# Attention and two MLPs in one program: pooled heads in pairs, two of VectorE's sums on GpSimd, and the attention's tasks at other places

## The reference

```python
def _attn_ref(q, k, v):                      # B, H, S, D = 4, 8, 576, 64
    q_d, k_d, v_d = means of q, k, v over each 4 rows         # 144 pooled rows
    out_d = sm_attn(q_d, k_d, v_d)           # softmax(q k / sqrt(D)) v, all 144 x 144
    out_up = np.repeat(out_d, 4, axis=2)
    mask = np.abs(pos[:, None] - pos[None, :]) < 4            # a band of 7 keys
    out_local = softmax(where(mask, q k / sqrt(D), -1e9)) v
    return out_up + out_local

x = attn.transpose(0, 2, 1, 3).reshape(2304, 512)
h = x @ w_in                                 # 512 x 2048
x = (maximum(h, 0) ** 2) @ w_out             # 2048 x 512
h = maximum(maximum(x @ w1, x @ w2), x @ w3) # 512 x 768 each
out = h @ w_out2                             # 768 x 512
```

## Time and profile before

| | |
|---|---|
| device time, median of 3 runs | 857.37 us (855.84 to 858.9) |
| profiled execution, device time | 856.62 us |
| its span | 854.9 us, mean granted clock 0.985 |
| TensorE matmul, weight load | 815.8 us (95%), 783.1 us (92%) |
| VectorE | 447.9 us (52%) |
| ScalarE | 331.6 us (39%) |
| GpSimd | 228.2 us (27%) |

### The profile page before, as it was taken

How to read it: one execution, slowest core, us unless ns; L and a number is a source line. 1 busy time by engine, 2 the same in 40 slices (tenths; PEclk the granted TensorE clock), 3 DMA queues, 4 the chain that set the end, 5 groups by cost and what they waited for, 6 DMA issues and landing times.

```text
span 854.9 us, 13859 instructions
## 1 busy us (share of the span) xinstructions
PE 815.8 (95%) x5701; PEld 783.1 (92%) x5701; DVE 447.9 (52%) x537; ACT 331.6 (39%) x908; POOL 228.2 (27%) x203
## 2 busy tenths in 40 slices
PE   8999979999989998999979999999999999999996
PEld 7888868999979998989979999999999999999996
DVE  5657856859977899767880008721222222122211
ACT  4685454464654454644635344211211112121111
POOL 8476911344411364332433222100000000000000
PEclk9999989999999998999999999999999999999998
...
GB/s 182 277 230 77 49 55 2 16 93 20 102 28 3 40 92 120 30 1 15 30 28 1 1 115 174 75 101 1 38 37 38 38 1 75 1 38 1 20 18 37
DMA packets 52752, 49.06 MB, mean 57 GB/s; under 512 B 23401, under 2 KB 44681, under 8 KB 51921
## 3 DMA queue, kind: packets, MB, share of 16 engines
...
## 4 chain that ended last, share of the span: by engine, by line
PE 75%; DVE 17%; ACT 3%; POOL 3%; issue 1%; POOLq 0%; DVEq 0%; ACTq 0%
PE PS L652 23%; PE PS L654 22%; PE PS L653 22%; DVE tmp L1308 4%; DVE qk L1320 3%; DVE tmp L1258 3%; DVE sc L1267 2%; PE PS L677 2%; PE PS L693 1%; PE PS L892 1%; ACT qkT L1029 1%; PE PS L684 1%; DVE prs L1344 1%; DVE prs L1342 1%; DVE qk L1337 1%
## 5 line engine op out<-in xcount | busy, mean ns | idle before, releaser
L652 PE MATMUL PS<-XS,WI 128*128 128x288 f32 (+1 forms) x768 | 244.2, 318 | 1.0 <-POOL WI L1716 1.0
L653 PE MATMUL PS<-XS,WI 128*128 128x288 f32 (+1 forms) x768 | 239.2, 311 | 0.0
L654 PE MATMUL PS<-XS,WI 128*128 128x288 f32 (+1 forms) x768 | 239.1, 311 | 0.0
L1736 POOL TENSOR_TENSOR G<-g,G 128x288 fp32r<-128x288 f32 x128 | 142.5, 1115 | 261.3 <-ACT G L1072 260.7
L652 PE MATMUL PS<-G,WO 128*128 128x288 f32 x512 | 158.0, 309 | 6.3 <-ACT x2s L1079 3.2
L653 PE MATMUL PS<-G,WO 128*128 128x288 f32 x512 | 152.6, 298 | 0.0
L654 PE MATMUL PS<-G,WO 128*128 128x288 f32 x512 | 152.2, 297 | 0.0
L652 PEld LDWEIGHTS PS<-XS,WI 128*128 128x128 f32 x768 | 145.3, 189 | 5.2 <-issue 2.1
L653 PEld LDWEIGHTS PS<-XS,WI 128*128 128x128 f32 x768 | 145.9, 190 | 1.3
L654 PEld LDWEIGHTS PS<-XS,WI 128*128 128x128 f32 x768 | 145.5, 189 | 0.0
L1067 ACT ACTIVATE PS<-PS 128x288 f32<-128x288 f32 x128 | 50.9, 398 | 153.7 <-PE PS L654 127.8
...
## 6 DMA issues: line engine op xcount, KB each, us to landing
x_scratch<-x2s SPq DMA_DIRECT2D x8, 576.0 KB, 4.0
...
qk<-q SPq DMA_DIRECT2D x6, 576.0 KB, 5.4
...
```

Of the source, the lines that this page charges most:

```text
L652: mm(dst, wt(HI), xt_(HI), start=first, stop=False)
L653: mm(dst, wt(HI), xt_(LO), start=False, stop=False)
L654: return mm(dst, wt(LO), xt_(HI), start=False, stop=last)
L1736: Q.tensor_tensor(G[:, s % NGR, LO], g32[:, s % 2], G[:, s % NGR, HI].bitcast(f32), ALU.subtract).then_inc(g_ready, 1)
```

## The change

- **Heads in pairs.** The tasks s, t and o now take two heads, c = 0 to 3. Both heads of a pair use the banks 6 and 7 side by side, one each (`heads_s`, `heads_o`), and all three kinds of task use both. s alternates between the partitions 0 to 63 and 64 to 127. s, t and o of a pair stand 0, 4 and 6 places behind its start, the pairs 8 places apart. VectorE's minimum (`heads_max`) takes a pair, ScalarE's copies too; its exps stay four a pair. `OD_PARTS` is now heads 0 to 5 and 6 to 7.
- **k and v sums.** Of batches 2 and 3 GpSimd makes them, one addition behind each of three G's, at the steps of `SUMS_AT`. k's load now waits for the sums of the batch before.
- **Batch 1.** Its three sums stand on VectorE's program ahead of the rest of the band scores, its qk tasks begin at (0, 14), its heads at (1, 1), beside the band scores.
- **Places.** qk tasks are three places apart in place of two; `QK_AT`, `HEADS_AT`, `X_AT`, `EXP_AT` and five entries of `SECOND_AT` differ. SP does `pooled_v_to_tokens(1)` ahead of `store_x2(0)`.
- **Weights.** VectorE makes the lo part of tiles 21, 25 and 29 too; tile 8 is split in step 2, tile 10 behind that step's square.
- **Opening.** GpSimd makes a 32x96 mask (`one_behind`) in place of the 32x2304 one and copies it to its place behind the sums; the load of `v_blk` no longer waits for it.

```diff
-    for n in range(NH + 4):
-        heads.append(([("o", n - 4)] if n >= 4 else []) + ([("s", n)] if n < NH else []))
-        heads.append([("t", n - 2)] if 2 <= n < NH + 2 else [])
+    QK_PACE, HEADS_PACE, HEAD_AT = 3, 8, (0, 4, 6)
+    for c in range(KC):
+        heads += [(HEADS_PACE * c + later, [(kind, c)]) for kind, later in zip("sto", HEAD_AT)]
-    QK_AT = {1: (1, 0, 1), 2: (2, 14, 1), 3: (4, 9, 1)}
-    HEADS_AT = {1: (1, 3, 0), 2: (3, 0, 1), 3: (4, 13, 0)}
-    X_AT = {1: [(1, 14, 0), (1, 14, 2), (1, 15, 0), (2, 9, 0), (2, 9, 2), (2, 10, 0)],
-            2: [(3, 13, 0), (3, 13, 2), (3, 14, 0), (4, 4, 0), (4, 4, 2), (4, 5, 0)],
-            3: [(5, 10, 1), (5, 11, 1), (5, 12, 1), (6, 2, 0), (6, 2, 2), (6, 3, 0)]}
+    QK_AT = {1: (0, 14, 1), 2: (2, 13, 3), 3: (4, 11, 1)}
+    HEADS_AT = {1: (1, 1, 0), 2: (2, 15, 3), 3: (4, 13, 1)}
+    X_AT = {1: [(1, 14, 3), (1, 15, 0), (1, 15, 1), (2, 9, 3), (2, 10, 1), (2, 10, 3)],
+            2: [(3, 13, 2), (3, 14, 0), (3, 14, 2), (4, 8, 1), (4, 8, 3), (4, 9, 1)],
+            3: [(5, 12, 1), (5, 13, 1), (5, 14, 1), (6, 9, 1), (6, 10, 1), (6, 11, 1)]}
...
-                 ((0, 5, 1), ("S", 4)), ((0, 6, 2), ("ps", 3)), ((0, 7, 1), ("P", 4)), ((0, 7, 2), ("pt", 3)),
-                 ((0, 7, 3), ("S", 5)), ((0, 9, 0), ("po", 2)), ((0, 9, 0), ("po", 3)), ((0, 10, 0), ("P", 5)),
-                 ((0, 11, 0), ("out", 3)), ((0, 11, 1), ("out", 4)), ((0, 11, 3), ("out", 5))]
-
-    EXP_AT = {(1, 1): 2, (2, 1): 3, (2, 15): 4, (3, 13): 5, (4, 11): 6, (5, 11): 7}
+                 ((0, 5, 1), ("S", 4)), ((0, 6, 2), ("ps", 3)), ((0, 7, 2), ("P", 4)), ((0, 7, 3), ("pt", 3)),
+                 ((0, 8, 0), ("S", 5)), ((0, 9, 0), ("po", 2)), ((0, 9, 0), ("po", 3)), ((0, 10, 1), ("P", 5)),
+                 ((0, 11, 1), ("out", 3)), ((0, 11, 2), ("out", 4)), ((0, 12, 0), ("out", 5))]
+
+    SUMS_AT = {(2, "k"): (2, 5), (2, "v"): (2, 12), (3, "k"): (4, 4), (3, "v"): (4, 9)}
+
+    EXP_AT = {(1, 3): 2, (2, 0): 3, (3, 1): 4, (3, 15): 5, (4, 15): 6, (5, 15): 7}
...
-    OD_PARTS = [(0, NH - 3), (NH - 3, NH)]
+    OD_PARTS = [(0, NH - 2), (NH - 2, NH)]
...
-    W_EARLY = [[], [], [], [8, 10]] + [[2 * s + 4] for s in range(4, NF - 2)] + [[], []]
-    W_LATE = [[1, 6], [3], [5]] + [[2 * s + 1] for s in range(3, NF)]
+    W_EARLY = [[], [], [8], []] + [[2 * s + 4] for s in range(4, NF - 2)] + [[], []]
+    W_LATE = [[1, 6], [3], [5, 10]] + [[2 * s + 1] for s in range(3, NF)]
...
-    W_DVE = [1, 3, 5, 9, 13, 17]
+    W_DVE = [1, 3, 5, 9, 13, 17, 21, 25, 29]
...
                     sp.wait_ge(k_read, b - 1)
+                    sp.wait_ge(pooled_qk, 2 * (b - 1))
                     load_k(b)
...
+    for e in range(2):
+        last = mm(heads_s[:, e, n], qkT[64 * e:64 * e + 64, 0, c, q_part(n)], qkT[64 * e:64 * e + 64, 1, c, :],
+                  start=True, stop=True)
...
             second_lo_part(3)
             second_lo_part(4)
-            run(seg, 1)
+            dve.wait_ge(unseen_copied, 4)
+            pool_k()
             second_lo_part(5)
-            dve.wait_ge(unseen_copied, 4)
+            pool_q(1)
+            next_w()
+            pool_v()
...
+                if b == 1:
+                    run(seg, 1)
+                    next_w()
+                    run(seg, 3)
+                    heads_max(b, 0)
+                    run(seg, 4)
+                    heads_max(b, 1)
+                    run(seg)
+                    softmax_in(lo)
+                    softmax_out(lo)
+                    seg = value_steps(lo, two)
+                    run(seg, 3)
+                    heads_max(b, 2)
+                    run(seg, 4)
+                    heads_max(b, 3)
+                    run(seg)
+                else:
...
+                    run(seg, 7)
+                    pool_q(b)
                     run(seg, 4)
...
+                    heads_max(b, 0)
+                    run(seg)
+                    softmax_in(lo)
+                    heads_max(b, 1)
+                    softmax_out(lo)
+                    seg = value_steps(lo, two)
+                    run(seg, 4)
+                    heads_max(b, 2)
+                    run(seg, 4)
+                    heads_max(b, 3)
+                    run(seg)
                 dve.wait_ge(q_loaded[1], 16 * b)
+                scale_pooled(b, 0)
                 seg = score_steps(hi, two)
...
+            def row_sum(b, which):
+                if which == "k":
+                    dst, rows, made, done = pqk[:, :, 1], k_rows(0, GL), k_sums, pooled_qk
+                    pool.wait_ge(k_loaded, 48 * b)
+                    filled(pool, b - 1, ("o", KC - 1))
+                else:
+                    dst, rows, made, done = pv_rows, vb[:, HALO:HALO + GL, :], v_sums, pooled_v
+                    pool.wait_ge(v_loaded, 48 * b)
+                    pool.wait_ge(od_loaded, OD_MOVES * (b - 1))
+                src = view(rows, "p (j t) d -> p t j d", t=POOL)
+                Q.tensor_tensor(dst, src[:, 0], src[:, 1], ALU.add).then_inc(made, 1)
+                yield
...
                 for place in range(1, PLACES):
                     x_lo_parts(s, place)
+                if s in row_sums:
+                    next(row_sums[s])
```

More of the change, by code:

```diff
@@ L1729, in x_lo_parts @@
                         x_lo_part(b, task[1])
+            for i in W_FIRST:
+                split_w(i)
+            def row_sum(b, which):
[10 more added lines that the diff above has]
+                yield
+                pool.wait_ge(made, 2 * (b - 2) + 1)
+                Q.tensor_tensor(dst, dst, src[:, 2], ALU.add).then_inc(made, 1)
+                yield
+                pool.wait_ge(made, 2 * (b - 2) + 2)
+                Q.tensor_tensor(dst, dst, src[:, 3], ALU.add).then_inc(done, 1)
+                yield
+            row_sums = {}
+            for (b, which), (n, f) in SUMS_AT.items():
+                additions = row_sum(b, which)
+                for i in range(POOL - 1):
+                    row_sums[NF * n + f + i] = additions
             for s in range(TOTAL):
```

156 lines of the change are left out of this document (67 added, 89 removed).

## The result

The changed kernel takes **836.0 us** (median of four executions, 828.2 to 836.6) against 858.1 for the kernel before: a ratio of 0.9725, 95% interval 0.966 to 0.979. The profiled execution took 836.6, with a span of 834.9. The forecast was 825, its range 813 to 838.

The account below looks back on a forecast made before the run. TensorE's stream, its waits and their half clock were taken to bound the kernel. 10.5 + 0.9 + 2.2 + 12.8 + 6.0 = 32.4 off 856.6 gives 824.2, plus 0.8 is 825 us; range 813 to 838.

Parts of the forecast that it names:

- Heads in pairs, 10.5 less: TensorE's attention tasks in the three later batches: 12 pairs at 2.5 us replace 24 heads at 1.68, 10.5 us less.
- rival 2: Inside each pair, TensorE waits 1.3 us for VectorE and ScalarE between scores and turn: 15.6 more, 840 us; chance 0.12.
- Opening, 0.9 less: Opening: smaller GpSimd masks remove the pooled scores' wait of 1.2 us; 0.9 less, between 0 and 1.2.
- Batch 0, 2.2 less: Batch 0: TensorE's waits of 1.0 us for GpSimd's WI and 1.2 on VectorE's x2s go; 2.2 less.
- Waits behind 100 us, 12.8 less: TensorE's waits after 100 us fall from 22.9 to 10.1 us, those before the x transposes going: 12.8 less.
- GpSimd's sums: Batches 2 and 3: twelve additions leave VectorE, freeing 12.4 us; 0.5 us put on each, within the margins.
- Rival 3: GpSimd's sums block VectorE through the shared port; TensorE waits 4 us before (4,8) and the clock falls: 832 us; chance 0.10.
- its two signs: VectorE's products at 2.5 us beside GpSimd's sums, and a TensorE wait before (4,8).
- Clock, 6.0 less: TensorE's half-clock stretches cost 2.5 us in place of 8.5, as waits up to 1.8 bring no fall: 6.0 less.
- Rival 1: TensorE's new waits behind 100 us don't come: 8 of 10.1 us and 2.5 of clock go, 814 us; chance 0.17.
- Rivals 2 and 4: The second of these: the wait at each pair's turn reaches 2.5 us and brings half clock, 872 us; chance 0.05.
- The forecast's own case: Whole kernel: 818 to 831 us, ends set by q's load, the opening and one clock window; chance 0.56.

Follow-up runs that it names:

- h2_pairs_dear: Changed kernel with the opening's wait filled (828.5 us), plus eight idle transposes ahead of each pair's outputs: 837.3 us.
- g4_pairs_only: Kernel before with the heads in pairs and nothing else, first output at its old place: 856.8 us, ratio 0.999.
- f3_vblk_waits: Changed kernel with v_blk's load held until both parts of the token rows v_tok have landed: 834.2 us.
- f4_series: Changed kernel with a pair's four score records reordered, both of partitions 0 to 63 first, then both of 64 to 127: 834.7 us.
- g1_sums_vector: Changed kernel with the opening's wait filled (828.5 us) and the k and v sums of batches 2 and 3 back on VectorE: 823.2 us.

## Why the prediction was right or wrong, point by point

- **Heads in pairs, 10.5 less.** Right in size: 0.84, 0.55 and 1.10 where I had 0.84, 0.55 and 1.1, 10.2 less on TensorE, 8.7 of it in the time (h2_pairs_dear). The danger that I named (rival 2, ScalarE and VectorE inside a pair) did not come: no turn or output waited. What I did not say is that it holds only beside the rest of the change; in the order before it is worth nothing (g4_pairs_only).
- **Opening, 0.9 less.** This step failed. It became 9.1 more, and it is most of what separates 836.0 from the forecast of 825: with the wait filled the kernel takes 828.5, so 7.5 of the 11 are this. I followed the removed wait to ScalarE's exps and VectorE, not to the next thing that GpSimd makes for TensorE, the v sums, whose token rows land at 16.2 whatever the masks cost. The two kernels' sums end at the same 24.4. The new wait of 1.45 at a place with little work then cost 8 us of clock. I had also put no price on the copy that moves behind the sums: beside it VectorE's product takes 2.74 in place of 1.02, and in the wait for it the clock fell in f3_vblk_waits and f4_series. My bounds of 0 to 1.2 held no clock at all, because I had counted half clock only behind 100 us.
- **Batch 0, 2.2 less.** 0.6 at step (0, 13) against (0, 0). The wait for WI went as I had it; of the 1.2 on VectorE's x2s 0.8 stayed, and 0.8 came new for a weight tile that VectorE now splits later.
- **Waits behind 100 us, 12.8 less.** 9.9 less. s(0) of the three batches: 0.07, 1.7 and 1.2 for qkT where I had 1.0, 2.1 and 1.9; x of batch 1 1.5 where I had 1.2. Mis-sized were three: the q rows, 5.0 for 3.0 (the rows could be summed 7.3 us behind their load's issue for 6.6, the sum took 3.9 for 2.9, and of the 3.5 that the rows themselves gave I had taken 3.0), batch 2's q sum, 1.5 where I had none, and the x transposes, 2.2 where I had none: VectorE's margin of 1.3 us ahead of (4, 8) was an overshoot of 0.9.
- **GpSimd's sums.** The reason of the last two of those three, and of part of the first: with the sums on VectorE the x transposes wait for nothing, batch 2's q sum 0.3, and batch 3's q rows still 3.7 (g1_sums_vector). I had put 0.5 us on each addition, 6 in all, against 12.4 freed. It was 12.6 against 12.5. The term mis-sized is the one that I bounded by the earlier trace rows, a product beside a G of 288 columns; a sum is longer, it collides with two or three instructions. Rival 3 had the mechanism, and a chance of 0.10; its two signs came, a VectorE product of 2.47 beside the sums and a wait of 0.9 ahead of (4, 8), and it cost 5.4 us in the measurement where the rival had 7.
- **Clock, 6.0 less.** 20.4 us at half clock became 6.8 behind 100 us, 5.5 of them outside the wait, which is the 2.5 that I took. The 20.5 of the opening are in its own point. The rule behind the term, that waits up to 1.8 bring no fall, did not hold: one of 1.45 brought it in the opening, and those of 1.6 to 1.7 at batch 2's scores did in four of eleven profiles.
- **Sum.** 10.2, 0.6, 9.9 and 6.0, less 9.1: 17.6 of the 20.0 by which the span shrank. The other 2.4 I have not broken down.
- **The rivals.** Rival 1 (the new waits don't come) was wrong: they came, larger. Rivals 2 and 4 were far off; no pair waited inside. The forecast's own case, 818 to 831, was missed from a side on which no rival stood, and that 836.0 lies within 813 to 838 is luck: what brought it there is in none of the terms.
